# Layernorm statistics in five GpSimd instructions, a new order of the attention stage, and later stores of the turned groups

## The reference

```python
# attention, per chunk of 32 queries (q_c), keys and values with 8 memory rows in front
scores = scale * np.matmul(q_c, k_full.transpose(0, 1, 3, 2))
a = np.exp(scores - np.max(scores, axis=-1, keepdims=True))
a = a / (np.sum(a, axis=-1, keepdims=True) + 1e-09)
out[:, :, c_start:c_end] = np.matmul(a, v_full)
# first feed-forward stage: x is 3072 x 512, w_in 512 x 1024, w_out 1024 x 512
h = x @ w_in
e = np.exp(h - np.max(h, axis=-1, keepdims=True))
solu = h * e / (np.sum(e, axis=-1, keepdims=True) + 1e-09)
mu = np.mean(solu, axis=-1, keepdims=True)
var = np.mean((solu - mu) ** 2, axis=-1, keepdims=True)
x = ((solu - mu) / np.sqrt(var + 1e-06) * g_ln) @ w_out
# second feed-forward stage: 512 -> 2048 -> 512
h = x @ w_in2
out = np.maximum(0.01 * h, h) @ w_out2
```

## Time and profile before

| | us |
|---|---|
| median of 3 runs | 860.04 (858.68 to 864.19) |
| the profiled execution | 860.89 |
| its span, from first to last instruction | 859.1 |
| PE busy | 812.4, 95% of the span |
| DVE, ACT, POOL busy | 545.1, 454.1, 114.2 |
| granted TensorE clock, mean | 0.986 of full speed |

### The profile page before, as it was taken

One profiled execution on the slowest core, in us unless ns is written; L12 is line 12 of the kernel. 1 busy time (PEld: TensorE's weight loads), 2 busy tenths in 40 slices (PEclk: granted clock), 3 DMA queues, 4 the chain that ended last, 5 costly groups with the idle time before them and its releaser, 6 DMA issues.

```text
span 859.1 us, 13067 instructions
## 1 busy us (share of the span) xinstructions
PE 812.4 (95%) x4860; PEld 661.9 (77%) x4860; DVE 545.1 (63%) x899; ACT 454.1 (53%) x729; POOL 114.2 (13%) x268
## 2 busy tenths in 40 slices
PE   8988889798939999999999999999989999999998
PEld 7766667686728888888888888888767888888886
DVE  6778788676742227452655243555678889769875
ACT  3567667574751334534556445656554554555443
POOL 3354546344330000000000000000000000000000
PEclk9999999899978999999999999999999999999999
DMA  9638675837339577724758467644780570174001
GB/s 338 214 131 238 214 193 176 244 132 190 74 100 274 191 264 252 244 98 172 240 201 295 147 211 257 220 170 159 279 296 25 199 266 26 51 269 146 26 1 73
DMA packets 79887, 156.63 MB, mean 182 GB/s; under 512 B 6224, under 2 KB 35024, under 8 KB 79824
## 3 DMA queue, kind: packets, MB, share of 16 engines
q1 hardware_dynamic: 79824, 155.81, 54.6%
HBM read 99.16 MB, written 56.62 MB: 181 GB/s over the span
## 4 chain that ended last, share of the span: by engine, by line
PE 67%; DVE 2%; DMA 2%; ACT 1%; issue 1%; POOL 1%; SPq 1%; POOLq 0%; ACTq 0%; DVEq 0%
PE hid_a L665 14%; PE hid_b L665 13%; PE scores_a L665 12%; PE attn_ps L665 12%; PE scores_b L665 8%; PE probs_ps L665 6%; DMA g_blk<-g_scratch 1%; DMA g_scratch<-g_out 1%; ACT u L830 1%; DVE ring_lo L1058 1%; DVE g_blk L1195 0%; ACT e L825 0%; DVE lnT L1116 0%; DVE u L1105 0%; SPq L525 0%
## 5 line engine op out<-in xcount | busy, mean ns | idle before, releaser
L791 ACT ACTIVATE ring_hi<-g_blk 128x512 fp32r<-128x512 f32 x168 | 105.9, 632 | 110.9 <-PE hid_b L665 40.7
L1058 DVE TENSOR_TENSOR ring_lo<-g_blk,ring_hi 128x512 fp32r<-128x512 f32 x168 | 115.5, 690 | 36.2 <-ACT ring_hi L791 33.0
L926 ACT ACTIVATE g_out<-g_out 128x512 f32<-128x512 f32 x72 | 45.4, 630 | 91.5 <-DVE g_out L1174 60.2
L1058 DVE TENSOR_TENSOR ln_op_lo<-ln_blk,ln_op_hi 128x512 fp32r<-128x512 f32 x48 | 32.4, 688 | 47.6 <-ACT ln_op_hi L791 47.6
L791 ACT ACTIVATE ln_op_hi<-ln_blk 128x512 fp32r<-128x512 f32 x48 | 29.7, 628 | 59.8 <-PE attn_ps L665 36.2
L665 PE MATMUL hid_b<-ring_hi,w_hi 128*128 128x512 f32 x128 | 50.3, 393 | 2.9 <-DVE ring_lo L1058 2.9
L665 PE MATMUL hid_b<-ring_hi,w_lo 128*128 128x512 f32 x128 | 49.9, 390 | 0.0
L830 ACT ACTIVATE u<-u,shift,gain 128x1024 f32<-128x1024 f32 x24 | 29.8, 1242 | 38.0 <-POOL shift L1353 38.0
L665 PE MATMUL hid_b<-ring_lo,w_hi 128*128 128x512 f32 x128 | 49.9, 390 | 0.0
L1116 DVE STREAM_TRANSPOSE lnT<-u 128x1024 f32<-128x1024 f32 x24 | 29.7, 1239 | 27.6 <-ACT u L830 27.6
L665 PE MATMUL hid_a<-w_in_hi,xT_hi 128*128 128x512 f32 x96 | 41.2, 429 | 4.8 <-DVE u L1105 2.8
(11 more groups left out here) (206 smaller groups left out, 2198.2 us busy)
## 6 DMA issues: line engine op xcount, KB each, us to landing
attn_buf<-kv_in SPq DMA_DIRECT2D x32, 768.0 KB, 5.5
g_scratch<-g_out SPq DMA_DIRECT2D x96, 256.0 KB, 2.4
g_blk<-g_scratch SPq DMA_DIRECT2D x48, 512.0 KB, 7.4
ln_scratch<-lnT SPq DMA_DIRECT2D x24, 512.0 KB, 7.6
ln_blk<-ln_scratch SPq DMA_DIRECT2D x24, 512.0 KB, 7.5
w_raw<-w_in SPq DMA_DIRECT2D x16, 512.0 KB, 4.4
q_raw<-q_in SPq DMA_DIRECT2D x32, 192.0 KB, 5.3
x_scratch<-x_stage SPq DMA_DIRECT2D x6, 1024.0 KB, 5.4
```

Of the source, the lines that this page charges most:

```text
L791: return act.activation(dst, src, ACT.Copy)
L926: act.activation(x, x, ACT.Prelu, alpha=0.01).then_inc(s_g[q], 1)
L1058: return ve.tensor_tensor(dst, x, hi.bitcast(f32), ALU.subtract)
```

## The change

`stats` is split in two. `stats_a` needs only `e_sum` and so stands as soon as `expo1` is done: floor = (1e-3 (e_sum + 1e-9))^2 in two instructions. `stats` then computes sq_sum / 1024 + floor, its power -0.5 as `gain`, and `shift1`: three instructions and one power where there were seven and two. Multiplying out, this is the same `gain` as before. A constant column and its memset go (the waits on `s_init` fall from 5 to 4), and `place_q` now waits for whatever `probs` and `stats` stand ahead of it. `START` and `BLOCK_STEPS` are written in a new order; and `store_ln` is put behind the second `load_attn` after the fourth `tr` of its group (in the last block, at once).

```diff
--- before.py
+++ after.py
@@ -104,69 +104,67 @@
 
 
 START = (
-        ("place_q", 0), ("place_q", 1), ("keep_warm", 12),
-        ("scores", 0), ("shift", 0), ("expo", 0), ("rsum", 0),
-        ("keep_warm", 8),
-        ("scores", 1), ("probs", 0), ("place_q", 2), ("shift", 1),
-        ("probs_t", 0), ("w1_hi", 0), ("spread", 0), ("w1_lo", 0), ("expo", 1), ("rsum", 1),
-        ("scores", 2), ("probs", 1), ("place_q", 3),
...
+        ("keep_warm", 12), ("place_q", 0),
+        ("scores", 0), ("keep_warm", 8), ("place_q", 1), ("shift", 0), ("expo", 0), ("rsum", 0),
+        ("scores", 1), ("probs", 0), ("shift", 1), ("w1_hi", 0),
+        ("probs_t", 0), ("place_q", 2), ("expo", 1), ("w1_lo", 0), ("spread", 0), ("rsum", 1),
+        ("values", 0), ("load_attn", 4), ("probs", 1),
+        ("scores", 2), ("x_hi", 0), ("x_lo", 0),
+        ("probs_t", 1), ("shift", 2), ("w1_hi", 1),
...
+        ("values", 4), ("load_attn", 8), ("load_w1", 5), ("neg_max", 1), ("expo", 6), ("stats_a", 0),
+        ("probs_t", 5),
+        ("scores", 7), ("x_hi", 4), ("solu", 0), ("spread", 5), ("expo1", 1), ("rsum", 6),
+        ("hidden", 2, 0), ("x_lo", 4), ("square", 0), ("probs", 6), ("shift", 7),
+        ("hidden", 2, 1), ("stats_a", 1), ("solu", 1), ("stats", 0),
...
 BLOCK_STEPS = (
-        ("scores", 4), ("x_hi", 2),
-        ("hidden", 0, 0), ("tr", -2), ("expo1", -1), ("shift", 4),
+        ("scores", 4), ("neg_max", -1), ("norm", -2), ("x_hi", 2),
+        ("hidden", 0, 0), ("shift", 4), ("x_lo", 2), ("expo1", -1),
         ("probs_t", 3),
-        ("hidden", 0, 1), ("spread", 3), ("x_lo", 2), ("expo", 4), ("solu", -1),
-        ("hidden", 0, 2),
-        ("values", 3), ("load_attn", 7), ("rsum", 4), ("square", -1),
-        ("scores", 5), ("probs", 4), ("place_q", 6), ("x_hi", 3),
-        ("hidden", 1, 0), ("stats", -1), ("shift", 5),
-        ("probs_t", 4), ("x_lo", 3), ("expo", 5), ("spread", 4),
-        ("hidden", 0, 3), ("rsum", 5), ("norm", -1), ("probs", 5), ("place_q", 7),
-        ("hidden", 1, 1), ("neg_max", 0), ("tr", -1),
+        ("hidden", 0, 1), ("solu", -1), ("expo", 4), ("stats_a", -1), ("spread", 3), ("place_q", 6),
+        ("hidden", 0, 2), ("tr", -2), ("rsum", 4), ("square", -1),
+        ("values", 3), ("load_attn", 7), ("probs", 4),
+        ("scores", 5), ("stats", -1), ("x_hi", 3),
+        ("hidden", 1, 0), ("shift", 5), ("x_lo", 3), ("norm", -1),
+        ("probs_t", 4), ("expo", 5),
+        ("hidden", 0, 3), ("spread", 4), ("place_q", 7), ("tr", -1), ("rsum", 5),
...
     add(*START)
 
 
+    waiting = []
     for t in range(1, BLOCKS + 1):
         for kind, offset, *rest in BLOCK_STEPS:
             if kind in OF_UNIT and t * HEAD_PAIRS + offset < UNITS:
@@ -192,7 +191,14 @@
             elif kind not in OF_UNIT and t * TILES + offset < NT:
                 add((kind, t * TILES + offset, *rest))
                 if kind == "tr" and (t * TILES + offset) % GROUP == GROUP - 1:
-                    add(("store_ln", (t * TILES + offset) // GROUP))
+                    waiting.append((t * TILES + offset) // GROUP)
+                    behind = 2
+                if t == BLOCKS and waiting:
+                    add(("store_ln", waiting.pop()))
+            if kind == "load_attn" and waiting:
+                behind -= 1
+                if behind == 0:
+                    add(("store_ln", waiting.pop()))
             if t <= 2 and (kind, offset) in (("expo", 5), ("expo", 7)):
                 i = KM + 2 * (t - 1) + (offset == 7)
...
     def column(name, i):
         return at(name, small + 672 + 4 * NT * i, [P, NT])
 
-    neg_max, e_sum, inv_sum, u_sum, neg_mean, sq_sum, var, rstd, gain, shift1 = (
+    neg_max, e_sum, floor, u_sum, neg_mean, sq_sum, var, gain, shift1 = (
         column(x, i) for i, x in enumerate(
-            ("neg_max", "e_sum", "inv_sum", "u_sum", "neg_mean", "sq_sum", "var", "rstd", "gain", "shift1")))
+            ("neg_max", "e_sum", "floor", "u_sum", "neg_mean", "sq_sum", "var", "gain", "shift1")))
     minus_half = at("minus_half", small + 672 + 4 * NT * 10, [P, 1])
-    minus_one = at("minus_one", small + 704 + 4 * NT * 10, [P, 1])
 
     q_raw = [at(f"q_raw{i}", (202 + 1.5 * i) * KB, [P, BLOCK]) for i in range(2)]
...
                 ve.memset(diag[i][:, :, :, :], 0.0).then_inc(s_init, 1)
             ve.memset(minus_half[:, :], -0.5).then_inc(s_init, 1)
-            ve.memset(minus_one[:, :], -1.0).then_inc(s_init, 1)
...
                 op.then_inc(s_pool, 1)
                 pool.wait_ge(s_pool, own[0])
 
+            placed_behind = [0, 0]
+
             def place_q(a):
                 pool.wait_ge(s_q_in[a % 2], 16 * (a // 2 + 1))
-                if a >= 2:
-                    pool.wait_ge(s_probs, a - 1)
+                if placed_behind[0]:
+                    pool.wait_ge(s_probs, placed_behind[0])
+                if placed_behind[1]:
+                    pool.wait_ge(s_stats, placed_behind[1])
                 if a >= SLOTS:
                     pool.wait_ge(s_scores, a - SLOTS + 1)
                 else:
@@ -1337,22 +1345,27 @@
                 view = prob[a % 2][:, :].rearrange("q (n k) -> q n k", k=WINDOW)
                 pool.tensor_tensor(view, view, sm[:, :].unsqueeze(2).to_broadcast([P, PAIRS, WINDOW]),
                                    ALU.mult).then_inc(s_probs, 1)
+                placed_behind[0] = a + 1
 
             def stats(n):
 
                 c = slice(n, n + 1)
                 if n == 0:
-                    pool.wait_ge(s_init, 5)
+                    pool.wait_ge(s_init, 4)
                 pool.wait_ge(s_square, n + 1)
-                then(pool.tensor_scalar(inv_sum[:, c], e_sum[:, c], 1e-9, 1.0, ALU.add, ALU.mult))
-                then(pool.tensor_tensor(inv_sum[:, c], inv_sum[:, c], minus_one[:, :], ALU.pow))
-                then(pool.tensor_scalar(var[:, c], sq_sum[:, c], inv_sum[:, c], inv_sum[:, c], ALU.mult, ALU.mult))
-                then(pool.tensor_scalar(var[:, c], var[:, c], 1.0 / D_FF1, 1e-6, ALU.mult, ALU.add))
-                then(pool.tensor_tensor(rstd[:, c], var[:, c], minus_half[:, :], ALU.pow))
-                then(pool.tensor_tensor(gain[:, c], rstd[:, c], inv_sum[:, c], ALU.mult))
+                then(pool.tensor_scalar(var[:, c], sq_sum[:, c], 1.0 / D_FF1, floor[:, c], ALU.mult, ALU.add))
+                then(pool.tensor_tensor(gain[:, c], var[:, c], minus_half[:, :], ALU.pow))
                 pool.tensor_tensor(shift1[:, c], gain[:, c], neg_mean[:, c], ALU.mult).then_inc(s_stats, 1)
-
-            run(dict(place_q=place_q, probs=probs, stats=stats))
+                placed_behind[1] = n + 1
+
+            def stats_a(n):
+
+                c = slice(n, n + 1)
+                pool.wait_ge(s_expo1, n + 1)
+                then(pool.tensor_scalar(floor[:, c], e_sum[:, c], 1e-9, 1e-3, ALU.add, ALU.mult))
+                then(pool.tensor_tensor(floor[:, c], floor[:, c], floor[:, c], ALU.mult))
+
+            run(dict(place_q=place_q, probs=probs, stats=stats, stats_a=stats_a))
 
 
 def attention_layout(q, k, v, mem_k, mem_v):
```

More of the change, by code:

```diff
@@ L134 @@
-        ("scores", 6), ("neg_max", 1), ("probs", 5), ("place_q", 7), ("x_hi", 4),
-        ("probs_t", 5), ("solu", 0), ("expo1", 1), ("shift", 6),
-        ("hidden", 2, 0), ("spread", 5), ("x_lo", 4),
-        ("hidden", 2, 1), ("expo", 6), ("solu", 1), ("square", 0),
-        ("values", 5), ("load_attn", 9), ("load_w1", 6), ("rsum", 6), ("square", 1), ("stats", 0),
-        ("scores", 7), ("x_hi", 5), ("shift", 7), ("probs", 6), ("place_q", 8), ("norm", 0), ("stats", 1),
-        ("probs_t", 6), ("x_lo", 5),
@@ L166 @@
+        ("hidden", 1, 2), ("stats_a", 0), ("solu", 0), ("shift", 6),
+        ("probs_t", 5), ("x_lo", 4),
+        ("hidden", 1, 3), ("square", 0), ("expo", 6), ("spread", 5), ("place_q", 8),
+        ("hidden", 2, 0), ("rsum", 6), ("neg_max", 1), ("stats", 0),
+        ("values", 5), ("load_attn", 9), ("probs", 6), ("expo1", 1),
+        ("scores", 7),
+        ("hidden", 2, 1), ("x_hi", 5), ("solu", 1), ("stats_a", 1), ("shift", 7), ("norm", 0),
         ("probs_t", 6),
-        ("hidden", 2, 2), ("x_lo", 5), ("spread", 6), ("stats", 1), ("tr", 0),
@@ L168 @@
-        ("hidden", 2, 3), ("expo", 7), ("rsum", 7),
-        ("values", 6), ("load_attn", 10), ("norm", 1), ("neg_max", 2), ("probs", 7), ("place_q", 9),
+        ("hidden", 2, 2), ("square", 1), ("x_lo", 5), ("expo", 7), ("place_q", 9), ("spread", 6),
+        ("hidden", 2, 3), ("tr", 0), ("rsum", 7), ("stats", 1),
+        ("values", 6), ("load_attn", 10), ("probs", 7),
 )
@@ L802, in spread @@
                 if a == 0:
-                    act.wait_ge(s_init, 5)
+                    act.wait_ge(s_init, 4)
                 if a >= 2:
```

57 lines of the change are left out of this document (25 added, 32 removed).

## The result

The changed kernel takes **853.59 us**, median of 7 runs (852.65 to 854.83), against 860.04 for the kernel before (858.68 to 864.19): ratio 0.992, 95% interval 0.9899 to 0.9941. That is 6.5 us faster where I had forecast 15, and 0.6 us outside my range. The profiled execution took 853.10, its span is 850.9 (859.1 before).

A forecast was written before the change was run, and what follows sets the result against it. PE, busy 95% of the span, was taken as the bound, leaving its idle and lower-clock time to win. Blocks -19.5 + 5.2 + 8.0 = -6.3, start -5.0, end -3.5: -14.8, so 845 us against the median; range 834 to 853.

The forecast's parts named there:

- start: Before the first block: first `hidden` some 2.4 us sooner, 2.26 us stall gone; -5.0 us, bounds -2.5 and -6.5.
- end: Border to the x2 stage: shorter statistics of the last three tiles in series; -3.5 us, bounds -1.5 and -4.5.
- stores: New places: late queries' copy blocks POOL's `probs` at units 14, 19, 24; 2.0, 2.0, 1.2, together +5.2 us, bounds 2 and 14.
- Rival C: Queries behind load and stores land 3 us later still, three times: +9, 854 us; chance 0.13.
- order of a block: Six blocks: late steps cost 1.1 us each, 0.7 more in the two splitting weights; +8.0 us, bounds 0 and 12.
- 6.1 us of old excess: Old blocks: 19.5 us excess less 13.4 for stores, from statistics ahead of `probs` and `tr` ahead of `x_lo`; replaced by +8.0.
- walk: Block steps followed with old-trace durations: `tr` waits for `norm`, hole stays empty, `values` 21 is 0.4 to 0.9 us late.
- Rival B: In the blocks, the new order costs PE nothing: +0 to 2 instead of +8.0, stores 3, 836 us; chance 0.27.
- D: In every block, `spread` behind `expo` is late in all four units: 36 in place of 8, 873 us; chance 0.05.
- E: At the end, shorter statistics don't shorten the chain: -1 instead of -3.5, 848 us; chance 0.05.

The follow-up runs named there:

- `stores_only`: The kernel before with the four stores of a group two loads later and nothing else: 849.15 us, ratio 0.9854.
- The eight combinations: ACT, DVE and POOL each on old or new block order, with short statistics, late stores, new start: all old 838.60, all new 853.59 us; DVE's alone costs 22.4.
- the late weight load: The changed kernel with the last weight load two loads later on SyncE, behind the load of unit 12: 851.93 us, ratio 0.9894.
- the transpose and the copy: The changed kernel with one transpose per block back behind `neg_max` and each copy of queries behind `probs` of the unit two before: 850.38 us, ratio 0.9880.
- `tr_behind`: The changed kernel with the transpose of tile 3t-1 back behind `neg_max` of tile 3t: 850.91 us, ratio 0.9874.

## Why the prediction was wrong

The **start** was right: -6.1 against -5.0. The first `hidden` began at 16.04 (forecast 16.6) and the 2.26 us stall is gone. In part this is luck: with the old `START` the short statistics alone already ended it at 55.56 instead of 57.61, and I had put their gain there at nothing, so the new start itself brought some 4 of the 6.1. (`stores_only`, which edits nothing there, ended it at 59.07, so a single profile may be off by 1.5 us.) What the start is worth at the end is less: with short statistics and late stores, it brings 1.4 us (839.95 to 838.60). In front of the old block order the stretch from `values` 3 to `values` 7 takes 25.28 us with the new start and 23.00 with the old one; in the changed kernel, 23.5.

The **end** was right: -3.9 against -3.5. The last tile's statistics take 245.62 - 244.46 = 1.2 us where they took 2.7:

```profile
244.46 0.26 POOL L1356 TENSOR_SCALAR var<-sq_sum,floor 128x1 f32<-128x1 f32 x1 [2.34 <-ACT e L830]
...
245.43 0.19 POOL L1358 TENSOR_TENSOR shift<-gain,neg_mean 128x1 f32<-128x1 f32 x1
```

I had taken off 1.0 us for the transpose of tile 20; with the old order and short statistics the stretch takes 24.27, so that move cost 0.1. I called the shorter statistics no gain inside a block. That was too low: in the experiment they bring 8.8 us in all, of which the stretch behind the last `values` has 4.1 (28.32 to 24.27), and PE's pace in the two free blocks went from 25.44 to 25.06.

The **stores** cost less than forecast in the changed kernel. The wait for keys and values is gone, as said. What they visibly leave on PE are the waits for `probs` of 1.09 and 0.63 us (units 19 and 24), against 5.2. That is not their price by themselves: where only POOL is on the new order, so that ACT and DVE are on time, the third and the fifth block, in which the copies of the queries behind the second and third store fall, take 29.16 and 26.01 us instead of 25.06, and the fourth, without such a copy, 25.07. In the changed kernel the same two blocks take only 1.0 and 0.7 us more than the fourth. The third block with POOL alone on the new order:

```profile
111.78:140.94 29.16, 25.58 (x277) 1.00 0.70 208
```

Rival C's number, 854, was hit, its mechanism not. SP and POOL of after at the third store and the copy of the queries issued behind it:

```profile
159.92 6.63 SPq L423 DMA_DIRECT2D ln_scratch<-lnT  x4
166.60 1.98 SPq L405 DMA_DIRECT2D q_raw<-q_in  x1
```
```profile
173.30 1.05 POOL L1338 COPY attn_buf<-q_raw 64x384 f32<-64x384 f32 x2 [4.16 <-DMA q_raw<-q_in]
```

The stores held SP for 6.63 us behind a load, 5.50 without (7.58 and 7.82 at the two earlier ones). But from the begin of the stores to the copy it took 13.4 us, where it took 13.0 (13.8 and 14.3 at the earlier ones): 0.4 to 1.3 us more, not 3. The Trainium skill (DMA: Bandwidth & Descriptors, "Queues, rings and completion order") says that each DMA engine consumes an issuing engine's descriptors in ring order. The trace agrees in sign, by these 0.4 to 1.3 us; that the 768 KB ahead would be added in full was rival C's price, not the page's, and that did not come.

**The failed step is the order of a block**: "I take 1.1 us a block over six blocks, and 0.7 more in the two with weights to split: +8.0", bounds 0 and 12, and with it that the 6.1 us of old excess "is replaced by this". Against the old order I had thus priced it, with 5.2 for the stores (mostly the copy ahead of `probs`), at 8.0 - 6.1 + 5.2 = 7, and it costs 15. The forecast by block, in its own terms (25.44, plus 1.1 or 1.8, plus 2.0, 2.0 and 1.2 for the stores in the second, third and fifth), beside the changed kernel and the same without the new block order:

```
block                first  second third  fourth fifth  sixth  sum
forecast             27.24  29.24  28.54  26.54  27.74  26.54  165.8
changed kernel       32.97  31.77  28.12  27.09  27.76  25.28  173.0
without new order    28.38  28.38  25.06  25.06  25.06  24.37  156.3
```

Of the miss of some 7.2 us, the first two blocks, those with weights, have 8.3; the other four are 1.1 us shorter than forecast. The sixth is so by an error of reading: I said that each stretch holds the same PE work, but the last has 254 matmuls and not 277, and its own pace is 24.4. In the undisturbed (fourth) block the walk was right in kind (the transpose waits for `norm`, the hole before `solu` stays empty, `spread` stands behind `expo`, PE waits 1.04 and 0.37 us), but against 25.06 it costs 2.0 instead of 1.1; 0.4 of that is that I took 25.44 for PE's own pace. The third and fifth came near the forecast because the dearer order and the cheaper stores cancelled. In the blocks with weights, the 2.9 that they have over 25.44 in the old order was not replaced, and 4.6 and 3.4 came on top of the 28.38, where I had 1.8 over 25.44 in each and 2.0 for the store in the second. I had priced each engine's move by itself, next to engines on time. The eight combinations show that this is what fails: the costs don't add. How it happens in these two blocks is read from the timelines and not shown by a run: `norm` ahead of `spread` and the weight piece on ACT, the low half ahead of `rsum` on DVE and the copy ahead of `probs` on POOL each add a wait for the next engine, and seem to close a loop. Undoing one link of it (the late weight load, -1.7 us), or two others (the transpose and the copy, -3.2), left most of the cost. **Rival B** (the new order costs nothing) fell. D (all four units late) did not come about; 14 waits in 24 units averaged 0.9 us. E fell, too.

The rest of the program, which I took at zero, has +1.1 us; over all runs it took 601.0 to 603.5 us without an edit, so this is scatter.

**What stays open.** The eight combinations show whose order costs what beside which others, and `tr_behind` names one move of DVE worth 2.0 us in a steady block and, beside the new orders of ACT and POOL, all that DVE's order costs. Which moves make the 22.4 us of DVE's order alone, and which of ACT's and POOL's make the 12 us that remain with the transpose back, above all in the blocks with weights, no run separates.

## What to carry to other kernels

Price a reordering over all engines at once. A step that waits is as dear as everything queued behind it, and if that queue holds what the releasing engine itself needs, a small lateness can run around the loop, as the timelines of the worst block suggest; so it is worth a try to put steps with a far releaser (statistics, queries, a split weight) behind those that feed the bounding engine, and a filler between a reduction and the step that waits for another engine's answer. Test such an order with each engine's part alone as well as undone: one engine put back among changed ones says what its order costs beside theirs (DVE 2.6 us), not what it costs alone (22.4). Undo the parts before reading a small gain as a small effect: here -21.6 and +15 hid in -6.5.
